# A routed-expert kernel: aligned stage buffers, eight gather buffers with the third expert fetched among them, and one-hot columns made contiguous

## What is computed

```python
# 1: causal attention in a window of 64, batch 4, 8 heads, 576 positions, head size 64
scores = where(0 <= pos_q - pos_k < 64, q @ k.T / 8, -1e9)
x = softmax(scores) @ v                      # then reshaped to x[2304, 512]
# 2: mixture of 8 experts, the best 2 for each of the 2304 tokens
noisy = x @ w_gate + log1p(exp(x @ w_noise)) * noise
top2 = the two largest of noisy[token];  top2_w = softmax over those two
out[mask] += top2_w * (relu(x[mask] @ w1[e]) @ w2[e])      # w1: 512x1024, w2: 1024x512
# 3: a dense layer
h = out @ w_in;  g = where(h >= 1, h, where(h <= -1, 0, (h + 1)**2 / 4));  y = g @ w_out
```

## Time and profile before

| | |
|---|---|
| time, median of three runs | 1140.97 us (1139.37 to 1141.7) |
| the profiled execution's own time | 1140.15 us |
| its span in the trace | 1138.6 us |
| TensorE busy | 1086.2 us, 95% |
| VectorE, ScalarE, GpSimd busy | 346.6, 351.7, 355.0 us |
| mean granted TensorE clock | 0.976 |
| moved by DMA | 121.96 MB |

### The profile page before, as it was taken

How to read it: one execution, slowest core, us unless ns; L and a number is a source line. 1 busy time by engine, 2 the same in 40 slices (tenths; PEclk the granted TensorE clock), 3 DMA queues, 4 the chain that set the end, 5 groups by cost and what they waited for, 6 DMA issues and landing times.

```text
span 1138.6 us, 19459 instructions
## 1 busy us (share of the span) xinstructions
PE 1086.2 (95%) x6597; PEld 928.5 (82%) x6598; DVE 346.6 (30%) x652; ACT 351.7 (31%) x797; POOL 355.0 (31%) x230
## 2 busy tenths in 40 slices
PE   7999489997699999999999999999999999999998
PEld 5998368886588888888888887889889899898896
DVE  5888621221011221121122112334132242241421
ACT  4676312121121222122222212425234143252441
POOL 3000067434882917345361803750110101101000
PEclk8999689999799999999999999999999999999999
DMA  9896355778353333324141422220110101101000
GB/s 233 222 228 158 121 176 185 229 256 288 96 181 111 120 120 111 111 92 147 53 169 55 140 73 65 91 77 10 55 40 15 55 0 55 46 9 55 8 12 19
DMA packets 68706, 121.96 MB, mean 107 GB/s; under 512 B 25728, under 2 KB 30976, under 8 KB 68160
## 3 DMA queue, kind: packets, MB, share of 16 engines
q0 software_dynamic: 16688, 62.66, 17.1%
q1 hardware_dynamic: 38496, 34.72, 11.0%
q10 hardware_dynamic: 13488, 24.12, 6.5%
HBM read 87.66 MB, written 33.82 MB: 107 GB/s over the span
## 4 chain that ended last, share of the span: by engine, by line
PE 81%; DMA 8%; POOL 7%; issue 2%; DVE 1%; SPq 0%; ACT 0%; POOLq 0%; DVEq 0%
PE bank L1115 6%; PE bank L1114 6%; PE bank L1113 6%; PE bank L1053 6%; PE bank L1051 6%; PE bank L1052 6%; PE bank L1036 5%; PE bank L1038 5%; PE bank L1037 5%; PE bank L1100 5%; PE bank L1099 5%; PE bank L1098 5%; POOL Wl L378 4%; DMA x_sorted<-gath 3%; DMA gath<-x_rows,token_of 3%; PE bank L924 3%
## 5 line engine op out<-in xcount | busy, mean ns | idle before, releaser
L378 POOL TENSOR_TENSOR Wl<-stage,Wh 128x2048 fp32r<-128x2048 f32 x36 | 165.8, 4606 | 3.0
L1098 PE MATMUL bank<-zT_h,Wh 128*128 128x256 f32 x576 | 161.9, 281 | 1.0 <-DVE zT_l L861 1.0
L1099 PE MATMUL bank<-zT_l,Wh 128*128 128x256 f32 x576 | 161.8, 281 | 0.0
L1100 PE MATMUL bank<-zT_h,Wl 128*128 128x256 f32 x576 | 161.7, 281 | 0.0
L1036 PE MATMUL bank<-Wh,xT_h 128*128 x344 | 141.1, 410 | 19.7 <-POOL Wl L378 18.1
L827 DVE COPY y_out<-bank 128x512 f32<-128x512 f32 x43 | 29.7, 691 | 393.1 <-PE bank L1053 393.1
L1038 PE MATMUL bank<-Wh,xT_l 128*128 x344 | 137.4, 399 | 0.0
L1037 PE MATMUL bank<-Wl,xT_h 128*128 x344 | 136.6, 397 | 0.0
L1053 PE MATMUL bank<-Wh,hT_l 128*128 x344 | 136.4, 397 | 0.0
L1051 PE MATMUL bank<-Wh,hT_h 128*128 x344 | 135.8, 395 | 0.2 <-issue 0.2
L1052 PE MATMUL bank<-Wl,hT_h 128*128 x344 | 135.3, 393 | 0.0
(11 more groups left out here) (156 smaller groups left out, 1656.7 us busy)
## 6 DMA issues: line engine op xcount, KB each, us to landing
stage<-w POOLq DMA_DIRECT2D x32, 1024.0 KB, 5.7
x_sorted<-gath SPq DMA_DIRECT2D x43, 256.0 KB, 4.0
y_sorted<-y_out ACTq DMA_DIRECT2D x43, 256.0 KB, 2.1
x_in<-x_sorted ACTq DMA_DIRECT2D x41, 256.0 KB, 2.7
x_rows<-x_blk SPq DMA_DIRECT2D x36, 128.0 KB, 3.6
out<-o_out SPq DMA_DIRECT2D x36, 128.0 KB, 2.3
q_bd<-qT SPq DMA_DIRECT2D x16, 256.0 KB, 4.9
stage<-w_in POOLq DMA_DIRECT2D x4, 1024.0 KB, 5.7
```

The lines of the kernel that those rows point to most:

```text
L378: nc.gpsimd.tensor_tensor(Wl[:, s, cols], stage[:, c % 2], Wh[:, s, cols], ALU.subtract).then_inc(w_ready, 1)
L1098: nc.tensor.matmul(here, high, zT_h[:, k], start=(k == 0), stop=False)
L1099: nc.tensor.matmul(here, high, zT_l[:, k], start=False, stop=False)
L1100: mm = nc.tensor.matmul(here, low, zT_h[:, k], start=False, stop=(k == KD - 1))
```

## The change

Four things are changed together.

1. A filler of 96 bytes stands ahead of the stage buffers. The first of them (`q_bd`, and `x_in` and `square`, which share its place) began at byte 170272 of each partition, 32 bytes past a multiple of 128; now all these buffers begin at 170368, a multiple of 128 that is not one of 256. `stage`, `Wh` and `Wl` lie ahead of the filler and stay where they were, on multiples of 128.
2. The ring has eight buffers (`GB`), and SP runs its bounces two ahead of its confirmations (`LAG`) where it ran one ahead.
3. Chunks 0 and 1 of the third expert (number 2) are fetched after `last_parts` of the second, ahead of gather 12. Later fetches stand behind the split of the expert before, which is where they fell already.
4. `oh_lo` is laid out with each column's 128 values side by side, and is made by 36 instructions of 128 elements (L804 of the changed kernel) from `io_lo` and a column of `lo_f`, in place of three of 1536 elements. ScalarE's helper `all_lo` goes.

```diff
+    GB, LAG = 8, 2
@@
+        sb("align", [P, 24])
@@
-            oh_lo = sb("oh_lo", [P, P, 2 * NT], BF16)
+            oh_lo = sb("oh_lo", [P, 2 * NT, P], BF16)
-            all_lo = sb("all_lo", [P, P, 2 * NT], BF16)
@@
-            gath = sb("gath", [P, 4, D])
+            gath_a = sb("gath_a", [P, GB // 2, D])
...
+            gath_b = sb("gath_b", [P, GB // 2, D])
+            def gath(r):
+                return gath_a[:, r] if r < GB // 2 else gath_b[:, r - GB // 2]
@@ SP
-            bounce(0, 0, 16)
-            with sp.Fori(0, (TILES - 1) // 4) as m:
-                for r in range(4):
-                    bounce(4 * m + r + 1, (r + 1) % 4, 16 * m + (32 if r == 3 else 16))
+            for t in range(LAG):
+                bounce(t, t, 16)
+            LOOPED = (TILES - LAG) // GB
+            with sp.Fori(0, LOOPED) as m:
+                for r in range(GB):
+                    at = (r + LAG) % GB
+                    bounce(GB * m + r + LAG, at, 16 * m + (16 if r + LAG < GB else 32))
                     confirm(r, 16 * m + 16)
@@ POOL
                 if t == 12:
                     last_parts(1, 1)
-                if t >= 4:
-                    pool.wait_ge(bounced_r[t % 4], 16 * (t // 4))
+                    fetch_first(2)
+                if t >= GB:
+                    pool.wait_ge(bounced_r[t % GB], 16 * (t // GB))
@@
+            def reload(m, n, s):
+                used = pool.value_load(last_tile[0:1, bass.ds(n - 2, 1)], min_val=1, max_val=TILES + 1)
+                hold(y_done, used)
+                first_parts(m, n, s)
+                last_parts(n, s)
@@
-            with pool.Fori(1, E // 2) as m:
+            with pool.Fori(1, E // 2 - 1) as m:
                 for s in range(2):
-                    ...
+                    reload(2 * m + s, 2 * m + s, s)
+                    fetch_first(2 * m + s + 1)
@@ ScalarE
-            nc.scalar.activation(all_lo[:], io_lo[:].unsqueeze(2).to_broadcast([P, P, 2 * NT]),
@@ VectorE
-            for c in range(0, 2 * NT, PART):
-                nc.vector.tensor_tensor(oh_lo[:, :, c:c + PART], all_lo[:, :, c:c + PART],
-                                        lo_row[:, :, c:c + PART].to_broadcast([P, P, PART]),
-                                        ALU.is_equal).then_inc(onehots, 1)
+            for c in range(2 * NT):
+                inst = nc.vector.tensor_scalar(oh_lo[:, c], io_lo[:], lo_col[:, c:c + 1], None, ALU.is_equal)
+                if c % PART == PART - 1:
+                    inst.then_inc(onehots, 1)
@@ TensorE
-                mm = nc.tensor.matmul(ID_ps[:, 0:2 * TILES], oh_lo[:, :, c],
+                mm = nc.tensor.matmul(ID_ps[:, 0:2 * TILES], oh_lo[:, c],
```

More of the change, by code:

```diff
@@ L222, in build @@
         w_ready, passed = sem("w_ready"), sem("passed")
-        gathered = [sem(f"gathered{r}") for r in range(4)]
-        bounced_r = [sem(f"bounced_r{r}") for r in range(4)]
+        gathered = [sem(f"gathered{r}") for r in range(GB)]
+        bounced_r = [sem(f"bounced_r{r}") for r in range(GB)]
         bounced = sem("bounced")
@@ L307, in confirm @@
                 sp.sem_inc(bounced, 1)
-            bounce(0, 0, 16)
-            with sp.Fori(0, (TILES - 1) // 4) as m:
-                for r in range(4):
-                    bounce(4 * m + r + 1, (r + 1) % 4, 16 * m + (32 if r == 3 else 16))
-                    confirm(r, 16 * m + 16)
[L314 to L317, removed]
+            for t in range(LAG):
[5 more added lines that the diff above has]
+                    bounce(GB * m + r + LAG, at, 16 * m + (16 if r + LAG < GB else 32))
+                    confirm(r, 16 * m + 16)
+            for t in range(GB * LOOPED + LAG, TILES):
+                bounce(t, t % GB, 16 * (t // GB) + 16)
+                confirm((t - LAG) % GB, 16 * ((t - LAG) // GB) + 16)
+            for t in range(TILES - LAG, TILES):
+                confirm(t % GB, 16 * (t // GB) + 16)
             def keep(u, count):
@@ L461, in _ @@
                     last_parts(1, 1)
-                if t >= 4:
-                    pool.wait_ge(bounced_r[t % 4], 16 * (t // 4))
-                if t in (4, 5):
-                    pool.wait_ge(xg_done, t - 3)
+                    fetch_first(2)
+                if t >= GB:
+                    pool.wait_ge(bounced_r[t % GB], 16 * (t // GB))
+                if GB <= t < GB + 2:
+                    pool.wait_ge(xg_done, t - GB + 1)
                 pool.indirect_dma_start(
-                    out=gath[:, t % 4], out_offset=None, in_=x_rows[:, :],
+                    out=gath(t % GB), out_offset=None, in_=x_rows[:, :],
                     in_offset=bass.IndirectOffsetOnAxis(ap=token_of[:, t:t + 1], axis=0),
-                ).then_inc(gathered[t % 4], 16)
+                ).then_inc(gathered[t % GB], 16)
+            def reload(m, n, s):
[3 more added lines that the diff above has]
+                last_parts(n, s)
             pool.wait_ge(tables_ready, 1)
-            with pool.Fori(1, E // 2) as m:
+            with pool.Fori(1, E // 2 - 1) as m:
                 for s in range(2):
[L475 to L484, removed]
+                    reload(2 * m + s, 2 * m + s, s)
+                    fetch_first(2 * m + s + 1)
+            for n in range(E - 2, E):
+                reload(n, n, n % 2)
+                fetch_first(n + 1 if n + 1 < E else "in")
+            reload("in", E, 0)
             fetch_first("out")
@@ L575, in _ @@
             act.wait_ge(const_ready, ALL_CONSTANTS)
-            nc.scalar.activation(all_hi[:], io_hi[:].unsqueeze(2).to_broadcast([P, TILES, 2 * NT]), ACT.Copy)
-            nc.scalar.activation(all_lo[:], io_lo[:].unsqueeze(2).to_broadcast([P, P, 2 * NT]),
+            nc.scalar.activation(all_hi[:], io_hi[:].unsqueeze(2).to_broadcast([P, TILES, 2 * NT]),
                                  ACT.Copy).then_inc(route_act, 1)
@@ L780, in _ @@
             then(nc.vector.tensor_copy(hi_b[:], slot_hi[:]))
-            then(nc.vector.tensor_copy(lo_b[:], slot_lo[:]))
+            then(nc.vector.tensor_copy(lo_f[:], slot_lo[:]))
             dve.wait_ge(route_act, 3)
             pairs = "p a t -> p (a t)"
-            hi_row, lo_row, t_row = (a[:].rearrange(pairs).unsqueeze(1) for a in (hi_b, lo_b, io_t))
+            hi_row, t_row = (a[:].rearrange(pairs).unsqueeze(1) for a in (hi_b, io_t))
+            lo_col = lo_f[:].rearrange(pairs)
             then(nc.vector.tensor_tensor(oh_hi[:], all_hi[:], hi_row.to_broadcast([P, TILES, 2 * NT]), ALU.is_equal))
@@ L1009, in x_rows_of @@
             def x_rows_of(t, u):
-                return x_in[:, u] if has(t, 2) else gath[:, u]
+                return x_in[:, u] if has(t, 2) else gath(u)
             def transpose_x(t, u, k):
```

4 lines of the change are left out of this document (2 added, 2 removed).

## The result

| | before | changed kernel |
|---|---|---|
| time, median | 1140.81 us (1139.37 to 1141.7, 4 runs) | 1113.28 us (1110.74 to 1113.99, 4 runs) |
| the profiled execution's own time, its span | 1140.15, 1138.6 us | 1113.99, 1112.3 us |
| mean granted TensorE clock | 0.976 | 0.98 |
| TensorE busy | 1086.2 us | 1074.6 us |

The ratio of the times is 0.9756, 95% interval 0.9737 to 0.9774: 27.5 us less.

What follows compares the result with a forecast made beforehand. It took TensorE, busy 95% of the span, as the bound, its longest wait being 17.39 us for POOL's `Wl`. Terms -18.9 + 1.5 + 0.5 - 1.2 = -18.1 took 1140.15 to 1122.0, forecast 1122.5 us, range 1117 to 1129.5.

Steps and rivals of the forecast that it cites:

- Alignment: DMA queues and q loads at the start: aligned buffers win nothing, taken as 0, bounds -4.2 and 0.
- The stall, -18.9: Third expert's split ends before TensorE needs it: the 17.39 us wait and 1.55 us slow start go, -18.9 us.
- the ring stays slow: Rival: last gather at 268 or later, stall of 5 to 9 us left, 1129 to 1133 us; chance 0.13.
- more gathers in flight slow the ring: Rival: POOL's gather ring slows, at 3.0 us per tile a stall 5 us longer, 1145 us; chance 0.03.
- Confirmation two behind, +1.5: ACT's fetch of tile 4 waits for gather 6, delaying tile 1's relu and TensorE behind it: +1.5 us.
- another 1.55: TensorE's gap behind ACT's late relu: 1.55 us more if it also drops the clock.
- Two more gathers, +0.5: Start of the ring: extra gathers share the DMA engines with the first bounces, +0.5 us, bounds 0 and 1.7.
- One-hot columns, -1.2: One-hot columns made by 36 small VectorE instructions, read by TensorE as contiguous weights: -1.2 us in the sum.
- Faster start: Rival: aligned loads of q at the start take away up to 4.2 us, 1118 us; chance 0.07.

Runs made afterwards that it cites:

- lag1: The changed kernel with SP's bounces one ahead of the confirmations instead of two; 1108.65 us, ratio 0.9737 to the kernel before.
- onehot_only: The kernel before with only the new one-hot columns; 1141.86 us, ratio 0.9998.
- offset96: The kernel before with a filler of 64 bytes, putting the stage buffers 96 bytes past a multiple of 128; 1141.98 us.
- ring_and_fetch: The changed kernel without the filler and with the one-hot columns of before; 1127.22 us, ratio 0.9884 to the kernel before.
- g64: The changed kernel with old one-hots, second expert's first split before gather 8, and 64 bytes ahead of all dense-stage buffers; 1107.91 us, ratio 0.9715 to the kernel before.

## Why the prediction was wrong

**The step that failed** is the one under *Alignment*, "Nothing to win there". It read only the DMA queues and the loads at the start, and there it was right: the queues of the changed kernel keep the shares of the earlier trace rows:

```profile
q0 software_dynamic: 16688, 62.66, 17.0%
...
q10 hardware_dynamic: 13488, 24.12, 6.7%
```

But the buffers that moved are also TensorE's operands, and the step never asked what TensorE does with them. The term was 0 with bounds of -4.2 and 0; it measured 42 x 0.26 + 9 x 0.32 = 13.8 us in the two traces, and 10.6 us alone, 6.6 to 14.6 by its interval. With it the forecast for the profiled execution would have been 1122.0 - 13.8 = 1108.2; the misses below (+4.8 on ScalarE, +0.8 by the clock of the first product, +2.2 for the one-hots, -0.2 for the stall) and a start 1.9 us earlier give 1113.9, and it took 1113.99. The range had no room for this: its terms reached down to 1140.15 - 20.9 = 1119.3 (the prediction writes 1118.5), and none of them was TensorE's own pace.

**The stall, -18.9.** Right: in the kernel before, the step from tile 9 to tile 10 took 308.15 - 276.53 = 31.62 us where an undisturbed one takes 12.51, so stall and slow start were 19.1. The ring was forecast at 310 GB/s with its last gather at 252 us; it moved 337 GB/s at a DMA share of 0.95 and issued it at 245.68, 6 us ahead. The rival that the ring stays slow is out. The rival by which more gathers in flight slow the ring is out as well, since it takes 1.75 us a gather.

**Confirmation two behind, +1.5.** The mechanism was right to a tenth: the fetch of tile 4 went out at 177.17, the relu started at 177.71 (forecast 177.3), and TensorE waited 1.57 us. What the step priced was only the first wait. TensorE's timeline in the changed kernel:

```profile
178.36 1.15 PE L1072 MATMUL bank<-ident,hid 128*128 128x128 f32 x8 [1.57 <-ACT hid L612]
179.35 0.60 PE L1033 MATMUL bank<-ident,x_in 128*128 128x128 f32 x4
182.50 0.49 PE L1049 MATMUL bank<-Wh,xT_h 128*128 x1 [2.55 <-DVE xT_l L831]
```

The profile puts the 2.55 us in front of tile 2's first product to `xT_l`. The program does not ask for it there: the low part that ends just before, at 181.57, is tile 3's, and tile 2's was made at 165.70. In `lag1` the same product starts at 177.99, 3.3 us before tile 3's `xT_l`:

```profile
177.99 0.47 PE L1049 MATMUL bank<-Wh,xT_h 128*128 x1
```

```profile
181.31 0.69 DVE L831 TENSOR_TENSOR xT_l<-bank,xT_h 128x512 fp32r<-128x512 f32 x1 [0.84 <-ACT xT_h L605]
```

So the name in the brackets is wrong. The code has at this place TensorE's entry into its loop over tiles and the register loads of a tile; whether they make the gap was not shown. That it comes with the hold and goes with it is shown by `lag1`, where no wait stands before that product. And behind the two gaps the granted clock was 0.84 and then 0.76, as the windows view shows (the last columns are the granted clock, DMA share and GB/s):

```profile
182.00:185.00 3.00, 2.50 (x9) 2.08 (x10) 0.00 (x0) 0.00 (x0) 3.00 (x2) 0.84 0.94 358
185.00:190.00 5.00, 5.00 (x18) 3.95 (x18) 0.00 (x0) 0.70 (x2) 4.92 (x2) 0.76 0.22 81
```

From 183.97 to 187.62 nine matmuls start, 3.65 us where nine by 0.227 would be 2.04: 1.6 us. The prediction had named this ("another 1.55") and left it out of the sum. The term was 6.3 us, by `lag1`.

**Two more gathers, +0.5.** From `token_of` to the first product it is 154.91 - 145.81 = 9.10 us, and was 155.26 - 146.74 = 8.52: +0.6. That is the size forecast, but it is not shown to come from the gathers: the same stretch took 8.24 to 8.79 us in the seven other kernels with four buffers and 8.48 to 9.38 in those with eight. Nor is the longer first product (8.01 us against 7.23, by the lower clock): with four buffers it took anything from 5.92 us (`onehot_only`) to 8.23 (`offset96`).

**One-hot columns, -1.2.** Wrong in sign. VectorE and TensorE in the changed kernel:

```profile
137.35 5.94 DVE L804 TENSOR_SCALAR oh_lo<-io_lo,lo_f 128x128 bf16<-128x128 bf16 x36
```

```profile
139.44 5.98 PE L1013 MATMUL bank<-id_cols,oh_lo 128*128 128x86 bf16 x36 [8.54 <-DVE oh_lo L804]
```

36 instructions take 5.94 us, 0.165 each. The -1.2 of the sum rested on 0.12 us each, the author's estimate, which no run shows. `id_cols`, the row with the same operation and types, is followed after 0.54 us with 1548 elements: a twelfth of the elements took almost a third of that time. And the matmuls take 5.98 us, as good as the 6.05 of before, though their weights are contiguous now. The loads themselves did get shorter (TensorE's loads by line, before and after: busy us, mean ns of one, idle before):

```profile
L1000 PEld LDWEIGHTS bank<-id_cols,oh_lo 128*128 128x128 bf16 x36 | 5.2, 147 | 8.1 <-DVE oh_lo L791 7.5
L1013 PEld LDWEIGHTS bank<-id_cols,oh_lo 128*128 128x128 bf16 x36 | 4.2, 125 | 10.0 <-DVE oh_lo L804 9.1
```

But from the first start to the last the matmuls still follow one another by 0.161 us where it was 0.163. The clock is not what sets them apart from the 0.076 of the rank matmuls: it was granted at 0.50 for all three (windows 131.49 to 133.00 and 140.30 to 146.40 us before, 139.44 to 145.50 after). One difference that is left is the rank matmuls' contiguous moving side, which the prediction had named; it was not tried. The whole is +1.0 us, inside the bounds (-2.0 to +1.2).

**Faster start.** TensorE waited 2.1 us for q and not 4.2, but with the old places it waited 3.3 (`onehot_only`) and 2.8 (`ring_and_fetch`), and 3.9 with new ones (`lag1`): this wait varies by itself, and no gain of the alignment is to be seen in it.

## What to carry to other kernels

Where a change moves buffers, ask of each engine that reads them, not of the DMAs alone; when TensorE is busy for 95% of the span, half a per cent of its pace (by an estimate, 5.4 of the 1086.2 us here) is worth more than most waits. Compare the period of an undisturbed tile in both traces before anything else: it tells in two rows whether the work itself changed. A wait in a queue is priced by everything behind it until the pipeline has its slack again, the clock included, and not by the first engine that stands still: here it was 6.3 us, where the first wait was 1.57.

## What the runs showed of the hardware that was not expected

In this kernel the place of TensorE's operands in SBUF set its pace. With 512 columns streamed in fp32r, matmuls follow one another in 0.233 us when the distance of the two operands' first bytes is 32 modulo 128, and in 0.227 when it is 0; tiles took 12.51 us at 32, 12.49 at 96, 12.31 at 64 and 12.25 at 0. Modulo 128 does not say it all: the 64 of the tiles is 192 modulo 256, where these matmuls take 0.229 us, and at 64 modulo 256 (`g64`) they take 0.233. With 256 columns the range is wider, 0.1200 to 0.1134 us, and it goes otherwise: best were both `gT` and `zT` at 192 modulo 256, and `zT` alone there gave 0.1178. Why the place of `gT`, which is no operand of that product, or of `y` or `o_out`, should count, was not found. For the dense stage only the table is shown, and no rule for it is claimed. The other surprise was that the bf16 columns laid side by side, where they had been 72 bytes apart, shortened TensorE's loads from 147 to 125 ns and the matmuls behind them hardly at all, from 0.163 to 0.161 us each.
